# Softmax-free attention and two expert layers on one core: when the attention's inverse denominators are taken, loaded and multiplied

## The reference, cut to what matters

```python
def phi(x):                                     # x: batch 4, heads 8, 576 rows, 64 wide
    proj = x @ w_phi                            # 128 features
    proj = proj - max(abs(proj), axis=-1)
    return concatenate([exp(proj), exp(-proj)])
q_p, k_p = phi(q), phi(k)
kv  = k_p^T @ v                                 # per head
z   = sum(k_p over rows)
num = q_p @ kv
den = q_p @ z + 1e-06
attn = num / den                                # x of the next layer, 2304 x 512
h = attn @ w_in ; g = h * clip(h + 3, 0, 6) / 6 ; y = g @ w_out
# then: 8 experts, each row goes to one by argmax of its logits
```

## Time and profile before

| | |
|---|---|
| runs | 879.75 us median of 3 (877.52 to 882.30) |
| profiled execution | 878.82 us, its span 877.2 us, mean TensorE clock 0.973 |
| busy | PE 94%, PEld 59%, DVE 65%, ACT 44%, POOL 23% |
| PEclk in 40 slices of 22 us | 9978999899, then 9 but for the last |
| attention's last matmuls end | 219.80 us |

### The profile page before, as it was taken

How to read it: one execution, slowest core, us unless ns; L and a number is a source line. 1 busy time by engine, 2 the same in 40 slices (tenths; PEclk the granted TensorE clock), 3 DMA queues, 4 the chain that set the end, 5 groups by cost and what they waited for, 6 DMA issues and landing times.

```text
span 877.2 us, 19424 instructions
## 1 busy us (share of the span) xinstructions
PE 827.3 (94%) x7122; PEld 521.7 (59%) x7123; DVE 574.3 (65%) x1156; ACT 389.4 (44%) x842; POOL 203.4 (23%) x217
## 2 busy tenths in 40 slices
PE   6988989998899999999999999999998999999995
PEld 5655656665455555555455555555776667777773
DVE  4757786788797888898898898863741435222221
ACT  5756666777265465465565565532310112111110
POOL 4444657788100001001001001001121222111100
PEclk9978999899999999999999999999999999999998
DMA  7465485652555576586665666575353661646620
GB/s 222 138 185 162 153 232 176 196 168 87 206 200 197 192 230 228 191 230 228 212 208 227 205 214 228 132 280 186 135 199 113 256 250 62 237 180 225 234 81 14
DMA packets 67453, 164.41 MB, mean 187 GB/s; under 512 B 28614, under 2 KB 32966, under 8 KB 60736
## 3 DMA queue, kind: packets, MB, share of 16 engines
q1 hardware_dynamic: 61472, 146.74, 49.8%
q0 software_dynamic: 5760, 16.80, 5.4%
q10 hardware_dynamic: 160, 0.07, 0.0%
HBM read 114.16 MB, written 47.55 MB: 184 GB/s over the span
## 4 chain that ended last, share of the span: by engine, by line
PE 67%; DVE 12%; DMA 8%; issue 5%; SPq 4%; ACT 2%; POOL 0%; DVEq 0%; POOLq 0%; ACTq 0%
PE ps L893 17%; PE ps L882 14%; PE ps L976 12%; PE ps L988 12%; DMA rec<-den_sb 3%; DMA arena<-split 3%; PE ps L742 3%; PE ps L798 2%; PE ps L770 2%; DVE arena L1537 2%; DVE u_mx L1510 1%; DVE y_words L1502 1%; PE ps L966 1%; DVE relu L1593 1%; DMA recs<-rec 1%
## 5 line engine op out<-in xcount | busy, mean ns | idle before, releaser
L882 PE MATMUL ps<-arena,w_in_sb 128*128 128x384 f16 x1152 | 200.9, 326 | 1.0 <-issue 1.0
L893 PE MATMUL ps<-w_out_sb,arena 128*128 128x512 f16 x576 | 172.5, 381 | 7.4 <-DVE stage L1598 7.4
L882 PEld LDWEIGHTS ps<-arena,w_in_sb 128*128 128x128 f16 x1152 | 112.3, 98 | 82.2 <-issue 1.3
L976 PE MATMUL ps<-x_t,arena 128*128 128x128 f16 x2112 | 123.1, 220 | 6.0 <-issue 4.0
L976 PEld LDWEIGHTS ps<-x_t,arena 128*128 128x128 f16 x2112 | 120.9, 99 | 10.0 <-issue 6.7
L1262 ACT ACTIVATE x_t<-ps 128x512 f16<-128x512 f32 x54 | 31.6, 596 | 206.2 <-PE ps L976 180.9
L988 PE MATMUL ps<-arena,x_t 128*128 128x512 f16 x528 | 117.9, 379 | 0.0
L893 PE MATMUL ps<-w_out_sb,stage 128*128 128x512 f16 x288 | 109.7, 381 | 0.0
L1092 ACT ACTIVATE arena<-ps,arena 128x128 f32<-128x128 f32 x288 | 79.6, 384 | 54.6 <-DVE arena L1287 52.6
L1234 ACT ACTIVATE arena<-relu 128x384 f16<-128x384 f32 x96 | 50.0, 521 | 112.8 <-DVE relu L1593 111.6
L893 PEld LDWEIGHTS ps<-w_out_sb,arena 128*128 128x128 f16 x576 | 56.1, 98 | 68.4 <-issue 11.0
(11 more groups left out here) (206 smaller groups left out, 948.1 us busy)
## 6 DMA issues: line engine op xcount, KB each, us to landing
arena<-split SPq DMA_DIRECT2D x36, 1024.0 KB, 6.9
arena<-in_moe_w SPq DMA_DIRECT2D x16, 2048.0 KB, 13.6
split<-arena SPq DMA_DIRECT2D x16, 2048.0 KB, 7.4
arena<-in_qkt SPq DMA_DIRECT2D x15, 576.0 KB, 5.2
stage<-in_moe_w_in SPq DMA_DIRECT2D x16, 512.0 KB, 5.2
stage<-in_moe_w_out SPq DMA_DIRECT2D x16, 512.0 KB, 6.2
x_t<-rows POOLq DMA_DIRECT2D x27, 257.0 KB, 3.0
y_words<-recs SPq DMA_DIRECT2D x32, 144.0 KB, 3.0
```

Source lines behind the costliest of these rows:

```text
L882: last = nc.tensor.matmul(ps[:, HB[f % GB], 0:BN], w_in_sb[:, lw, c, f * P:(f + 1) * P], xt[:, a, lx, c, :], start=c == 0 and lw + lx == 0 ...
L893: last = nc.tensor.matmul(ps[:, YB + r, :], g_sb[lg_][:, f % GB, r * P:(r + 1) * P], w_out_sb[:, lw, f, :], start=f == 0 and lg_ + lw == 0 ...
L976: last = nc.tensor.matmul(ps[:, bank, f % 4 * P:(f % 4 + 1) * P], w1_sb[b][:, lw, c, f * P:(f + 1) * P], xgt[:, a, lx, c, :], start=c == 0 ...
```

## The change

The addition of 1e-6 leaves `reciprocals` and goes into the two copies of the denominators (a constant tile `tiny` is the bias on ACT). DVE takes the reciprocals of pair u - 2 in `pair_out(u)`. SP stores and loads the inverses of pair u - 3 in iteration u, in an attention loop of 16 iterations instead of 17; GpSimd multiplies pair u - 5 (its loop is written out). The last products, of pairs 11 to 15, are DVE's in block 0: 11 and 12 at f == 1, with the reciprocals of pairs 14 and 15 behind them; 13 and 14 at f == 4; 15 at f == 14. The two first unit loads now go out before rec_out(13), rec_in(13), den_over(15), and the rest of pairs 14 and 15. k's maxima are negated by a tensor_reduce over one element with `negate`. The first block's rows are split in two halves of the feature chunks, so that x_lo's first half can start after x_hi's first half. x_hi of block 1 waits for the first eight pairs instead of all.

```diff
@@ -37,7 +37,7 @@
-REP, WIDE = 32, 4
+REP, WIDE, BEHIND = 32, 4, 5
@@ SP: the inverses' way @@
             def den_over(u):
                 sp.wait_ge(low_copied, u + 1)
                 sp.wait_ge(high_copied, u + 1)
+                if u > 1:
+                    sp.wait_ge(rec_stored, (u - 2) * 16 + 16)
                 sp.dma_start(rec[:, u % 2, :], den_sb[0:P:REP, u % 2, :].rearrange("g (i t) -> g i t", t=PT)).then_inc(den_moved, 16)

             def rec_in(u):
                 sp.wait_ge(rec_stored, u * 16 + 16)
                 if u > 1:
                     sp.wait_ge(rec_loaded[u % 2], u // 2 * 32)
-                if u >= WIDE:
+                if u - WIDE > PAIRS - 1 - BEHIND:
+                    sp.wait_ge(x_last, u - WIDE - (PAIRS - 1 - BEHIND))
+                elif u >= WIDE:
                     sp.wait_ge(x_ready, u - WIDE + 1)
...
             next_qk(2)
-            for u in range(PAIRS + 1):
-                if u > 1:
-                    rec_out(u - 2)
+            for u in range(PAIRS):
+                if u > 2:
+                    rec_out(u - 3)
                 if u + 2 < PAIRS:
                     next_v(u + 2)
-                if u > 1:
-                    rec_in(u - 2)
+                if u > 2:
+                    rec_in(u - 3)
                 if 0 < u < PAIRS - 1:
                     next_pieces(u - 1)
                 if u > 0:
...
             sp.wait_ge(num_done, PAIRS)
             for m in range(2):
                 load_unit(0, m, m)
-            rec_out(PAIRS - 1)
-            rec_in(PAIRS - 1)
+            rec_out(PAIRS - 3)
+            rec_in(PAIRS - 3)
+            den_over(PAIRS - 1)
+            for u in range(PAIRS - 2, PAIRS):
+                rec_out(u)
+                rec_in(u)
@@ GpSimd @@
+            step(nc.gpsimd.memset(tiny[:], 1e-6))
...
-                if not isinstance(u, int) or u >= WIDE:
-                    normalise(u - WIDE, a)
+                if u >= BEHIND:
+                    normalise(u - BEHIND, 1 - a)
                 sums_first(u + 1)

             def last_pair():
                 sums_second(PAIRS - 1)
                 piece_hi_of(PAIRS - 1, 1)
-                normalise(PAIRS - 1 - WIDE, 1)
+                normalise(PAIRS - 1 - BEHIND, 0)
...
-            for u in range(1, WIDE):
+            for u in range(1, PAIRS // 2):
                 both(u, u % 2, 0)
-            with pool.Fori(WIDE // 2, PAIRS // 4) as i:
-                both(i * 2, 0, 0)
-                both(i * 2 + 1, 1, 0)
@@ ScalarE @@
-                nc.scalar.copy(den_sb[:, a, 0:QUARTER], ps[:, NB, DEN_AT:DEN_AT + QUARTER]).then_inc(low_copied, 1)
+                nc.scalar.activation(den_sb[:, a, 0:QUARTER], ps[:, NB, DEN_AT:DEN_AT + QUARTER], ACT.Identity,
+                                     bias=tiny[:, 0:1]).then_inc(low_copied, 1)

             def x_hi(n, b):
...
-                    act.wait_ge(x_ready, PAIRS - WIDE)
-                    act.wait_ge(x_last, WIDE)
-                nc.scalar.activation(xt[:, b, 0], x_t[:, :, bass.ds(n * BN, BN)], ACT.Copy, scale=s_up[:, 3:4]).then_inc(xs_hi, 1)
+                    first = isinstance(n, int) and n == 1
+                    act.wait_ge(x_ready, 2 * DC if first else PAIRS - BEHIND)
+                    if not first:
+                        act.wait_ge(x_last, BEHIND)
+                if isinstance(n, int) and n == 0:
+                    nc.scalar.activation(xt[:, b, 0, 0:2], x_t[:, 0:2, 0:BN], ACT.Copy, scale=s_up[:, 3:4]).then_inc(xs_half, 1)
+                    nc.scalar.activation(xt[:, b, 0, 2:DC], x_t[:, 2:DC, 0:BN], ACT.Copy, scale=s_up[:, 3:4]).then_inc(xs_hi, 1)
+                else:
+                    nc.scalar.activation(xt[:, b, 0], x_t[:, :, bass.ds(n * BN, BN)], ACT.Copy, scale=s_up[:, 3:4]).then_inc(xs_hi, 1)
@@ VectorE @@
-                nc.vector.tensor_scalar(k_neg[:, t0:t0 + n], mx[:, 2 * j, t0:t0 + n], -1.0, None, ALU.mult).then_inc(neg_ready, 1)
+                nc.vector.tensor_reduce(k_neg[:, t0:t0 + n], mx[:, 2 * j, t0:t0 + n, None], AX.X, ALU.max, negate=True).then_inc(neg_ready, 1)
...
-                nc.vector.tensor_copy(den_sb[:, a, QUARTER:2 * QUARTER], ps[:, NB + 1, DEN_AT:DEN_AT + QUARTER])
+                nc.vector.tensor_scalar(den_sb[:, a, QUARTER:2 * QUARTER], ps[:, NB + 1, DEN_AT:DEN_AT + QUARTER], 1e-6, None, ALU.add)
...
             def reciprocals(u, a):
                 dve.wait_ge(den_moved, u * 16 + 16)
-                nc.vector.tensor_scalar(rec[:, a, :], rec[:, a, :], 1e-6, None, ALU.add).then_inc(den_step, 1)
-                dve.wait_ge(den_step, u + 1)
                 nc.vector.reciprocal(rec[:, a, :], rec[:, a, :]).then_inc(rec_made, 1)

             def pair_out(u, a):
                 copy_high(u, a)
-                if not isinstance(u, int) or u > 0:
-                    reciprocals(u - 1, 1 - a)
+                if not isinstance(u, int) or u > 1:
+                    reciprocals(u - 2, a)
...
-                x_lo(0, 0)
+                first_x_lo()
...
+            def first_x_lo():
+                for k, hi in ((0, xs_half), (2, xs_hi)):
+                    dve.wait_ge(hi, 1)
+                    last = nc.vector.scalar_tensor_tensor(out=xt[:, 0, 1, k:k + 2], in0=x_t[:, k:k + 2, 0:BN], scalar=s_up[:, 3:4],
+                                                          in1=xt[:, 0, 0, k:k + 2], op0=ALU.mult, op1=ALU.subtract)
+                last.then_inc(xs_lo, 1)
...
                     if f == 0 and not post:
                         last_pieces()
-                        reciprocals(PAIRS - 1, 1)
-                    if 2 <= f < 2 + WIDE and not post:
-                        normalise(PAIRS - WIDE + f - 2, f % 2)
+                    if f == 1 and not post:
+                        normalise(PAIRS - 5, 1)
+                        normalise(PAIRS - 4, 0)
+                        for u in range(PAIRS - 2, PAIRS):
+                            reciprocals(u, u % 2)
+                    if f == 4 and not post:
+                        normalise(PAIRS - 3, 1)
+                        normalise(PAIRS - 2, 0)
+                    if f == 14 and not post:
+                        normalise(PAIRS - 1, 1)
```

More of the change, by code:

```diff
@@ L95, in moe_program @@
         three = sb("three", [P, 1])
+        tiny = sb("tiny", [P, 1])
         ones = sb("ones", [P, P])
@@ L251, in moe_program @@
         den_moved = sem("den_moved")
-        den_step = sem("den_step")
         rec_made = sem("rec_made")
@@ L279, in moe_program @@
         u_stored = sem("u_stored")
+        xs_half = sem("xs_half")
         xs_hi = sem("xs_hi")
```

## The result

The changed kernel takes 855.45 us (median of 4 runs, 853.36 to 858.78) against 880.37 of the kernel before in the same comparison: a ratio of 0.972, with a 95% interval of 0.968 to 0.977. The profiled execution took 853.36 us with a span of 851.8 us, 25.4 us less than the 877.2 of before. I predicted 858.5 us, within 846 to 873. Ratios leave out runs of a kernel that are over 1.5% above its fastest, so that a ratio need not be the quotient of two medians.

A forecast was written before the change was run, and what follows sets the result against it. The prediction took the kernel as PE-bound (PE busy 94% of the span). Its terms summed as 878.82 - 27 + 6.3 - 0.2 = 857.9 us for the profiled execution; median 858.5, own range 852 to 864, widened to 846 to 873.

The forecast's parts named there:

- Inverses two pairs behind: Attention: DVE's six waits for rec<-den_sb go, with PE's idle time and half clock; 27 us gained, 24 to 30.
- what I left to single pairs: Attention, excess kept: 1.0, 1.2 and 1.0 us in the scale pairs, 0.2 each in four others of the second half.
- rival C: Attention: another wait, ACT's for the den move, replaces the removed one; half the 27 us gained, 872 us; chance 0.15.
- Operations: Attention: 1e-6 added in the copies, negation by a reduce; 1 us credited to the negation, all inside the 27.
- First rows in halves: Start of block 0: x_lo can start without its 0.26 us wait for x_hi; 0.2 us gained.
- Unit loads moved up: Attention's end and block 0: small DMAs land behind 4 MB, DVE stands some 6.4 us; 6.3 us lost, 4 to 8.
- Later blocks: After block 0's start: products at f == 4 and f == 14 find their inverses; no time gained or lost.
- B: Block 0: the small DMAs pass the unit loads, no stall, and the old stall goes too; 848 us; chance 0.15.
- D: ACT in attention: Identity forces activation table reloads, 2.57 us per pair; slower, 897 us; chance 0.03.
- E: Block 0 stalls with no gain in attention, SP's queue taking up the freed time; 885 us; chance 0.02.

The follow-up runs named there:

- e2: The changed kernel with the old small operations put back (tensor_scalar negation, plain denominator copies, 1e-6 added before the reciprocal): 856.36 us, ratio 0.973 to the kernel before.
- e1: The kernel before with only the small operations changed (negation by tensor_reduce, 1e-6 added in the two copies): 873.17 us, ratio 0.994.
- e5: The kernel before with only the two first unit loads moved up to the attention's end: 882.6 us, ratio 1.008.
- e6: As e3, with the products of pairs 13 and 14 at f == 6 instead of f == 4: 849.71 us.
- e3: The changed kernel with rec_out(13) and den_over(15) issued ahead of the two first unit loads: 851.52 us, ratio 0.968 to the kernel before.

## Why the prediction was right

**Inverses two pairs behind** (27 us, bounds 24 and 30): 24.8 us from the second pair to T (196.53 to 171.74). Mechanism and place were right: no DVE wait, the clock stayed up, T at 194.0 where I had put it near 193. Of what I left to single pairs, the three with the scales have 12.69, 12.12 and 12.19 us, 1.67, 1.10 and 1.17 above 11.02 (I left 1.0, 1.2, 1.0). Two terms were too small, and I counted four other pairs in the second half where there are five. The pair at 113.15 kept 4.05 us, where I had left 0.2: there rival C took place once, ACT standing for the den move, because eight stores in SP's queue pushed it back; I had counted SP's queue as free between rec_in and den_over and not looked at iteration 7. The landing of recs<-rec, 1.6 us in the median before, is 3.8 now: the queue is fuller with every pair short, as I had feared for C, but the slack of a pair covers it elsewhere. And three of the plain pairs of the second half kept 0.42 to 0.56 us each, with ACT waiting for GpSimd's sums.

**Operations**: one less in the inverse and a faster negation, credited with about 1 us inside the 27; no gain that can be told with the lag in place (e2). ACT's Identity with a bias tensor took 403 ns in the median (386 to 415) where the copy had 302: my 0.30 was 0.1 low, beside PE.

**First rows in halves** (0.2 us gained): wrong in sign. It costs 0.93 us at the start of block 0. The step took the wait of 0.26 us for x_hi as what could be saved and didn't ask what stood ready on GpSimd to take the port between the halves. The 2.72 us of GpSimd's product before, where those of the pairs before took 1.41, were in the trace of before and would have told.

**Unit loads moved up** (6.3 us lost, 4 to 8): 5.4 us (tail 67.52 to 72.94). DVE's wait was 5.66 us for 6.4 predicted, PE's resumption T + 21.34 for T + 22.0. den_over(15) landed at T + 17.9, where I had T + 18; DVE came to it at T + 12.2 instead of T + 11.6. The clock cost about what I took: the 5.30 us behind the resumption ran at 0.50, and another 0.3 us behind them, so some 2.8 us were lost against 1.5 before, the difference 1.3 for my 1.5. That this term fitted is in part luck, since the half clock behind the same stall lasted 3.1 to 5.8 us from one profile to another.

```profile
215.36:220.66 5.30, 5.30 (x14) 2.00 (x15) 5.20 (x10) 1.61 (x3) 0.46 (x1) 0.50 0.15 56
```

**Later blocks**: nothing, as said; from block 0's copies to block 5's it is 324.59 us before and 324.69 after.

**What wasn't in the sum**: the expert stage took 265.3 us before and 260.2 after, 5.1 us less, with no edit in it. 1.8 us of it are PE's clock (248.21 us busy against 246.45), the rest is idle time. Most of it lies at one place, where PE, by the chain, waits for two loads of expert weights (arena<-split) before 96 matmuls of L976, now L983. Before, these loads took 14.3 us of the chain, PE was idle for 3.96 us and the 96 ran in 7.15 us, partly at half clock; after, they took 12.0, PE was idle for 2.14 and the 96 ran in 5.53. Of the twelve other profiles, six have half clock at that place and take 263.1 to 265.1 us for the stage (e1 and e5, with the attention of before, among them), and six don't and take 259.6 to 261.9. The two groups don't go with the edits: e6 has 264.6, e3 260.2. What makes those loads late in one execution and not in another stays open.

**How the sum came out**: against the 857.9 us forecast for the profiled execution, which took 853.36, the attention gained 2.2 us less, the tail lost 0.7 less (5.4 us for the 6.1 of the sum), the start was 1.0 shorter and the expert stage 5.1. The last two, which I hadn't foreseen, are why the measured time lies below the forecast; without them it would have been some 1.5 us above.

**Rivals**: B fell with e3 and e5: the small DMA did stand behind the 4 MB, 11.8 us in both e5 and the changed kernel. C came true in one pair. D fell: the trace has one table load, as before. E fell with the attention's 24.8 us.

## What to carry to other kernels

A wait of two or three microseconds for a small DMA can cost twice its length when PE falls idle behind it and its clock drops; ask for the result one iteration later before shortening the operations around it. In a queue, put the 4.5 KB that someone waits for ahead of the megabytes that nobody needs yet, and look for every burst of stores that stands in the same queue. When a shared resource is contended, two half operations let the other engine in between.

## What the runs showed of the hardware

- The store recs<-rec (4.5 KB, SP's queue) took 1.4 to 1.7 us to land at best, and 11.3 to 12.5 behind two loads of 2 MB, in each of the nine profiles that have it there (12.0 before, 11.8 in the changed kernel and e5). Its median rose from 1.6 us before to 3.8 in the changed kernel, whose pairs are shorter.
- A tensor_reduce of at most four elements took 153 to 159 ns in all 48 places of the changed kernel, 37 of them beside a GpSimd instruction. Of the tensor_scalar's 48 in the kernel before, 16 took 380 to 1104 ns, and all of these lie beside one (so do 17 of the 32 short ones).
- One x_lo of 128x1536 took 1.82 us with GpSimd's product held up behind it (2.72 us); two of 128x768 took 3.09 us with the product (1.57 us) in between.
